# The low parts of two weight pieces, made by POOL behind its last attention store and no longer by DVE

## The reference

```python
x = attention(q, k, v)                        # 1536 tokens x 512
logits = x @ w_gate
noisy = logits + log1p(exp(x @ w_noise)) * noise
top2 = argpartition(-noisy, 2)[:, :2]         # two experts per token, softmax weights
for e in range(8):
    out[mask] += top2_w * (relu(x[mask] @ w1[e]) @ w2[e])     # 512 -> 1024 -> 512
# then a second mixture: e_idx = argmax(logits), skipped where x @ w_skip <= 0
```

## Time and profile before

| | |
|---|---|
| time, median of 3 runs | 659.44 us (658.72 to 664.74) |
| the profiled execution | 660.48 us, its span 658.3 us |
| PE busy | 613.6 us, 93% of the span |
| DVE busy | 372.0 us, 57% |
| ACT busy | 292.0 us, 44% |
| POOL busy | 221.9 us, 34% |
| chain that ended last, by engine | PE 83%, DMA 6%, issue 4%, DVE 3%, POOL 1%, ACT 1% |
| L1613 (low parts of the first expert) | 8 on DVE |
| L1363 (high parts of the first expert) | 8 on POOL |

### The profile page before, as it was taken

One profiled execution on the slowest core, in us unless ns is written; L12 is line 12 of the kernel. 1 busy time (PEld: TensorE's weight loads), 2 busy tenths in 40 slices (PEclk: granted clock), 3 DMA queues, 4 the chain that ended last, 5 costly groups with the idle time before them and its releaser, 6 DMA issues.

```text
span 658.3 us, 13524 instructions
## 1 busy us (share of the span) xinstructions
PE 613.6 (93%) x4048; PEld 545.9 (83%) x4048; DVE 372.0 (57%) x706; ACT 292.0 (44%) x529; POOL 221.9 (34%) x223
## 2 busy tenths in 40 slices
PE   6888848999999999999999999995799999999994
PEld 6577735999999999999999999983588887888883
DVE  5779985544636445354543646336365587656641
ACT  2657733432524334343532534332365475635621
POOL 2558302204517054270623607214112222231230
PEclk9999966999999999999999999999699999999998
DMA  9999881452826629264382732808595679568220
GB/s 310 338 292 293 303 296 53 127 183 55 240 80 148 193 56 291 58 166 152 101 259 54 207 103 59 218 19 238 187 335 177 193 233 355 159 191 261 40 50 13
DMA packets 53105, 116.65 MB, mean 177 GB/s; under 512 B 10596, under 2 KB 10980, under 8 KB 53040
## 3 DMA queue, kind: packets, MB, share of 16 engines
q1 hardware_dynamic: 37728, 91.45, 41.4%
q0 software_dynamic: 11488, 23.93, 16.9%
q10 hardware_dynamic: 3824, 0.49, 0.5%
HBM read 100.36 MB, written 20.35 MB: 183 GB/s over the span
## 4 chain that ended last, share of the span: by engine, by line
PE 83%; DMA 6%; issue 4%; DVE 3%; POOL 1%; ACT 1%; SPq 1%; POOLq 1%; DVEq 0%; ACTq 0%
PE bank L871 22%; PE bank L865 22%; PE bank L980 21%; PE bank L854 2%; PE bank L834 2%; PE bank L748 2%; PE bank L727 2%; PE bank L996 2%; DMA v_raw<-in_v 2%; PE bank L761 2%; PE bank L716 2%; DMA out<-y_sb,ix_put 1%; DMA x_moe<-rows_out,ix_put 1%; PE bank L677 1%; PE bank L952 1%
## 5 line engine op out<-in xcount | busy, mean ns | idle before, releaser
L1605 DVE TENSOR_TENSOR w_lo<-stage,w_hi x120 | 141.6, 1221 | 22.7 <-ACT w_hi L1101 21.8
L1101 ACT CAST w_hi<-stage x120 | 119.7, 1049 | 9.0 <-PE bank L980 8.9
L871 PE MATMUL bank<-unit_hi,w_hi 128*128 128x416 f32 x256 | 92.6, 362 | 0.0
L1867 DVE SCALAR_TENSOR_TENSOR unit_lo<-bank,unit_hi 128x416 fp32r<-128x416 f32 x64 | 37.8, 591 | 96.7 <-ACT unit_hi L1208 96.7
L865 PE MATMUL bank<-tok_hi,w_hi 128*128 128x416 f32 x256 | 90.5, 354 | 0.6 <-DVE tok_lo L1819 0.6
L1208 ACT ACTIVATE unit_hi<-bank 128x416 fp32r<-128x416 f32 x64 | 33.1, 518 | 130.0 <-PE bank L865 130.0
L871 PE MATMUL bank<-unit_lo,w_hi 128*128 128x416 f32 x256 | 90.2, 352 | 0.0
L865 PE MATMUL bank<-tok_hi,w_lo 128*128 128x416 f32 x256 | 89.7, 350 | 0.0
L871 PE MATMUL bank<-unit_hi,w_lo 128*128 128x416 f32 x256 | 89.7, 350 | 0.0
L1431 POOL DMA_INDIRECT x_moe<-rows_out,ix_put x32 | 59.2, 1851 | 9.8 <-issue 9.8
L865 PE MATMUL bank<-tok_lo,w_hi 128*128 128x416 f32 x256 | 58.5, 350 | 0.0
(11 more groups left out here) (165 smaller groups left out, 1060.1 us busy)
## 6 DMA issues: line engine op xcount, KB each, us to landing
stage<-in_moe_w SPq DMA_DIRECT2D x128, 512.0 KB, 5.7
v_win<-in_v SPq DMA_DIRECT2D x24, 198.0 KB, 9.6
v_raw<-in_v SPq DMA_DIRECT2D x6, 528.0 KB, 13.3
x_moe<-rows_out SPq DMA_DIRECT2D x12, 260.0 KB, 3.9
kt<-in_k SPq DMA_DIRECT2D x8, 384.0 KB, 9.1
q_ring<-in_q SPq DMA_DIRECT2D x6, 512.0 KB, 10.2
x_att<-x_sb POOLq DMA_DIRECT2D x12, 256.0 KB, 6.1
stage<-x_moe SPq DMA_DIRECT2D x6, 512.0 KB, 6.6
```

The costliest lines, as they stand in the source:

```text
L871: last = eng.matmul(ps_out[chunk][:, 0:W], w[:, WC // 2 + f, chunk * P:(chunk + 1) * P], h[:, f % UNITS, :], start=(f == 0 and i == 0), st ...
L1101: eng.copy(piece(w_hi[n % SETS], j), stage[:, j, :]).then_inc(s_hi, 1)
L1605: eng.tensor_tensor(piece(w_lo[n % SETS], j), stage[:, j, :], piece(w_hi[n % SETS], j).bitcast(F32), ALU.subtract)\
L1867: eng.scalar_tensor_tensor(unit_lo[:, f % UNITS, :], ps_unit[f % 2][:, 0:W], 0.0, unit_hi[:, f % UNITS, :].bitcast(F32), ALU.max, ALU.subt ...
```

## The change

The low parts of pieces 6 and 7 of the first expert are no longer made by DVE in steps 24 and 25, but by POOL, behind its stores of tiles 10 and 11, on a semaphore of their own (`s_first_pool`). The three waits are divided accordingly: SP's loads of the next expert's pieces 6 and 7 wait for the new semaphore, and PE waits for six on the one and two on the other before its first `columns`.

```diff
+        POOL_SPLITS = (6, 7)
...
             def load_piece(g):
                 n, j = divmod(g, PIECES)
-                if n == 1:
+                if n == 1 and j < POOL_SPLITS[0]:
                     eng.wait_ge(s_first, j + 1)
+                elif n == 1:
+                    eng.wait_ge(s_first_pool, j - POOL_SPLITS[0] + 1)
...
                             if e == 0:
-                                eng.wait_ge(s_first, PIECES)
+                                eng.wait_ge(s_first, POOL_SPLITS[0])
+                                eng.wait_ge(s_first_pool, len(POOL_SPLITS))
...
             for t in (NT - 2, NT - 1):
                 store_x(t)
+            for j in POOL_SPLITS:
+                eng.wait_ge(s_fhi, j + 1)
+                eng.tensor_tensor(piece(w_lo[0], j), stage[:, j, :], piece(w_hi[0], j).bitcast(F32),
+                                  ALU.subtract).then_inc(s_first_pool, 1)
...
-            SPLIT_AT = (13, 15, 17, 19, 21, 23, 24, 25)
+            SPLIT_AT = (13, 15, 17, 19, 21, 23)
```

## The result

| | before | changed |
|---|---|---|
| time, median of 7 runs each | 660.88 us (658.72 to 664.74) | 666.20 us (663.05 to 670.11) |
| ratio | 1 | 1.0078, 95% interval 1.0055 to 1.0101 |
| the profiled execution | 660.48 us, span 658.3 us | 666.47 us, span 664.6 us |

The changed kernel is slower by about 5 us (0.0078 x 660.9 = 5.2 us, interval 3.6 to 6.7). The prediction said 661.1 us with a range up to 663.9 us, so the time lies outside it.

What follows compares the result with a forecast made beforehand. PE holds 83% of the chain of waits, which leaves it in routing. 0.0 (removed) + 1.7 (DVE behind POOL) + 0.0 (queues) + 0.0 (clock) = +1.7 us on 659.44 us: 661.1 us, range 659.3 to 663.9 us.

Steps and rivals of the forecast that it cites:

- DVE's relief: Ahead of tile 11's normalising: taking two subtractions off DVE only lengthens its wait for PE's products, gain 0.0 us.
- POOL's two subtractions last 4.65 us: Behind POOL's last store: two subtractions of 2.36 us each, joined closely, occupy POOL from about 86.5 to 91.15 us.
- DVE's two-input products can't run beside them: In the ranking: DVE's second product of two SBUF tensors, at 89.35 us, waits for POOL's subtractions, +1.7 us.
- So such an instruction stands until POOL's whole run is over: DVE beside POOL: drawn from earlier rows, it put the second product's end at 91.24 us instead of 89.53 us.
- the first of its instances, the cast at 37.23 us: Earlier in attention: DVE's cast took 2.58 us instead of 0.29 us, ending 0.09 us behind POOL's sum.
- so it goes first and POOL waits about 0.1 us: Start of the ranking: DVE's first product, at 86.28 us, begins 0.13 us ahead of POOL's subtractions and precedes them.
- The rival "the whole ranking waits": First ranking on DVE: POOL starts ahead of the first product, or searches stand too; +4.0 to +4.5 us, chance 0.13.
- POOL's store is issued 0.13 us faster: Start of the ranking: condition for the whole ranking to wait, or else ACT as much later.
- The queues: SP's loads of pieces 6 and 7 and PE's new wait: semaphores met 1.0, 0.65 and 33 us ahead, 0 us.
- The clock: PE's clock around the later fillers: taken as 0, with bounds of -0.5 us and at most +2.0 us.
- The chance of 0.97 for within 1%: Whole time: change within 1% (6.6 us) of before 0.97, faster by more 0.01, slower by more 0.02.

Runs made afterwards that it cites:

- e3: Changed kernel, but POOL fills the two pieces with zeros and reads nothing; ratio 1.0004, 18.67 us from the ranking's first product to the fillers.
- e2: Changed kernel, but POOL makes only piece 7's low part and DVE piece 6's; ratio 1.0078, 20.68 us from the first product to the fillers.
- e7: Changed kernel, but POOL's two subtractions wait until DVE begins the lists; ratio 1.0055, 22.46 us from the first product to the fillers.
- e1: Changed kernel, but POOL's subtractions wait on a semaphore until DVE's first ranking product is complete; ratio 1.0042, 20.41 us to the fillers.
- e10: Changed kernel with a POOL fill of 160 elements per partition ahead of its subtractions; first product 5.07 us, 23.14 us to the fillers.
- e13: Changed kernel with a 64-element POOL fill and POOL's own semaphore wait ahead of its subtractions; first product 0.24 us, 20.48 us to the fillers.
- e4: Changed kernel, but both POOL subtractions stand between its stores of tiles 10 and 11; ratio 1.0020, 18.94 us to the fillers.
- e9: Changed kernel with a POOL fill of 64 elements per partition ahead of its subtractions; first product 4.99 us, 23.06 us to the fillers.
- e12: Changed kernel, but POOL makes only piece 7's low part, between its stores of tiles 10 and 11; 18.31 us from first product to fillers.
- e11: Kernel before, with POOL's casts ahead of the store in each tile and the last casts moved to earlier tiles; ratio 0.9985.

## Why the prediction was wrong

- **DVE's relief is worth 0.0 us: right.** DVE idled 2.93 us ahead of tile 11's normalising (3.0 forecast), and e3 put the relief at 1.0004 (0.9969 to 1.0039; in the trace 18.67 us against 18.66).
- **POOL's two subtractions last 4.65 us: right.** 4.64 us, each 2.34 to 2.36 us.
- **DVE's two-input products can't run beside them: right** (e2, e3). "So such an instruction stands until POOL's whole run is over" was drawn too wide: it held for the two casts and the two subtractions, but in the same trace DVE's subtraction of 56.65 us was over 1.06 us ahead of the end of POOL's copies. And the first of its instances, the cast at 37.23 us, reads one tensor and not two; e7 shows that such instructions can be among those that stand.
- **"so it goes first and POOL waits about 0.1 us": this step failed.** It took the 0.13 us between recorded starts for the order in which the two get the port. The first product stood for 4.90 us although it is recorded as starting 0.15 us ahead. e1 shows that the rest of the working was sound where the product does go first (20.41 us against the 20.4 us that it gives), and e10 and e13 show that the recorded starts don't decide: at 0.32 us the product still stood, and with a wait of POOL's own ahead of the subtraction it did not. The reading that fits them is that POOL already had the subtraction in hand while its store was being issued; that is argued from these runs, and the hand-over itself is in no trace.
- **The rival "the whole ranking waits" is what happened**, at +4.31 us against the +4.5 us worked out for it. Its place was right; its turning point was not, "POOL's store is issued 0.13 us faster": no such shift was needed. It had a chance of 0.13 because I saw a margin where there was none. Its figure of 663.9 us missed the median too, since seven runs put the kernel before at 660.88 us and not at 659.44: 660.88 + 4.31 = 665.2 us, and 666.2 was measured. The rest of 1.0 us is within the interval of the ratio.
- **The queues: harmless, with margins that did not exist.** SP's loads of pieces 6 and 7 did wait for POOL, as this view of SP's waits in the changed kernel from 85 to 100 us shows (in all, times, longest):

```profile
SPq L579 <- POOL w_lo L1390: 1.7, 2, 1.4
```

  The forecast had them go unhindered; nobody needed the pieces, so it cost nothing. PE's new wait cost nothing.
- **The clock: 0, as taken.** From the fillers to the first expert's first product it took 121.22 - 111.19 = 10.03 us, against 115.01 - 104.94 = 10.07 us. In e4 and e9 it was 9.4 and 9.5 us, near the bound of -0.5 us; the longest of all was 10.10 us (e3). What the working did not look at is the clock ahead of the ranking, which fell to 0.50 before the last logits in some executions and not in others (0.3 us, see e12) and for 3.4 us in attention in the changed kernel's.
- **The chance of 0.97 for within 1%**: the ratio of 1.0078 lies within, with an interval that reaches 1.0101. The range was too low.

## What to carry to other kernels

Before work moves from VectorE to GpSimd, list VectorE's next instructions with two SBUF inputs, and those with one input and a scalar on fp16 tensors in SBUF. However short they are, those on the chain can stand for the reading instruction that GpSimd has in hand, and here stood for two casts or two subtractions in a row as well. A margin of a few tenths of a microsecond between recorded starts is none; if VectorE's instruction has to go first, let GpSimd wait on a semaphore for it, or put GpSimd's work where VectorE has no such instruction (between the stores here, 0.3 us instead of 4.3). Look for instructions that take longer than their like in the trace: here 1.80 and 2.78 us instead of 1.22 pointed at a gain that lay beside the change.

## What the runs showed of the hardware that was not expected

- A GpSimd subtraction recorded as starting 0.32 us behind a VectorE product (e10) still held it, though the product needs 0.24 us; with a semaphore of GpSimd's own ahead of the subtraction it did not (e13). Filling SBUF in the same place (1.86 us for two pieces) held nothing (e3).
- A VectorE subtraction that starts 0.29 us ahead of a GpSimd cast's recorded start can also go first (e11, 66.19 us). It had begun 0.25 us behind the start of GpSimd's store and not 0.41 us.
- VectorE's tensor-scalar instructions on 128 fp16 elements stood 2.33 us beside GpSimd's subtractions (e7), and one slipped in between two of them, which the product of two fp32 tensors did not in the changed kernel. A subtraction of two fp32 tensors got in between GpSimd's cast and the copies behind it, and between two copies (e11, before). Why the ones could and the others could not stays open.
